# The last four token tiles' picks of the first two routing rounds, on GpSimd instead of VectorE

## The chip, the cores and the metric

The program runs on one core of a Trainium2 chip. The metric is the device time of one execution in microseconds, from the first instruction of the core to its end. TensorE (PE in the rows) multiplies matrices, VectorE (DVE), ScalarE (ACT) and GpSimd (POOL) work on elements, and SyncE (SP) issues most of the large transfers.

## The reference, cut to what matters

Three stages follow each other: a windowed attention with sink keys, a mixture of experts with a capacity, and a dense feed-forward. The change lies in the second. Cut to it:

```
N, D, E, F = (1536, 512, 8, 1024)
cap = N // E                                  # 192 tokens for each expert
logits = x @ w_gate
order = np.argsort(-logits.flatten())
for idx in order:                             # best (token, expert) pairs first
    tok, e = (int(idx) // E, int(idx) % E)
    if assigned[tok] >= 0 or counts[e] >= cap:
        continue
    assigned[tok] = e
    counts[e] += 1
for e in range(E):
    mask = assigned == e
    h = np.maximum(x[mask] @ w1[e], 0.0)
    out[mask] = h @ w2[e]
```

After it every token runs through `g = max(x @ w_in, 0) + alpha * min(x @ w_in, 0)` and `g @ w_out`.

## The kernel before

The 1536 tokens lie as 12 tiles of 128 (`NT` is 12). The sequential loop of the reference is worked off in eight routing rounds. Each round finds the next expert that becomes full, with all 192 of its tokens. Round `r` goes like this. PE and VectorE rank the keys (`beats`, `ties`, `count`); VectorE takes the tokens in front of the filling one (`assign`), which raises `round_done`; PE counts for each token how many stand before it (`before_and_loads`); VectorE works out in `fill_expert` which expert is full and, for each token, its number among that expert's tokens (`slot`, one column for each token tile, 0 for a token that is not in it).

Then come the picks, the step of this study. For each token tile `c` one instruction writes `in_slot[:, c, :]`, 128 partitions by 192 numbers of 16 bits: 1 where `slot_iota` (1 to 192) equals the token's slot, else 0. It reads `slot_iota` as its tensor and `slot[:, c]` as one number for each partition. PE multiplies these one-hot tiles with the token numbers (`pick_tokens`): for each tile one matmul for 128 of the 192 slots and one for the other 64, 24 matmuls of one column in all. They are issued in two parts, `PARTS`, first tiles 0 to 7 (16 matmuls), then tiles 8 to 11 (8 matmuls), and each part waits for the picks of its tiles (`picks_ready`). `token_numbers` copies the result into `tok_next` on VectorE, and GpSimd gathers the 192 token rows with two indirect transfers (`gather`).

The order on each engine is the order in which its program is written. Around the picks it is:

- Round 0: nothing of the experts runs yet. VectorE does `assign(0)`, `fill_expert(0)`, 12 picks, `token_numbers(0)`, and then the key of the next round (`wanted_key(1)`). PE issues multiplications of zeros between its routing steps (`keep_clock`, 14 of them before `pick_tokens(0)` and 4 behind it), and then `rows(1, c)`, which waits for the key. The copies of ScalarE and the comparisons of VectorE of round 1 hang on that.
- Round 1: PE multiplies expert 0's tokens at the same time. `pick_tokens(1)` stands behind the second of the four output blocks of that expert. VectorE does 8 picks, `y_rest(0, 0)`, 4 picks, `token_numbers(1)`, `wanted_key(2)`.
- GpSimd has nothing to do between the attention's end and `gather(0)`, and nothing between `gather(0)` and `gather(1)`, other than one memset of a single number (`awake`), which waits for the first part of the picks. After that it splits `w_in` for the feed-forward (`split_wi`, `wi_lo`).

Later rounds (2 to 7) run beside the feed-forward or the experts and aren't touched by the change, but for the threshold that PE waits for.

Of the kernel before, what the change touches and what calls it, by code (L numbers as in the profile page):

```python
# [22 lines left out]
ALU = mybir.AluOpType  # L23
ACT = mybir.ActivationFunctionType
AX = mybir.AxisListType.X
# [33 lines left out]
def program(nc, q_t, k_t, k_sink, v_rows, v_sink_d, wg_d, w1_d, w2_d, w_in_d, w_out_d, alpha_d, out, n_sink, window):  # L59
# [9 lines left out]
    with ctx:  # L69
        def sb(name, shape, dt=F32, at=None):  # L70
            return (at or ctx).enter_context(nc.sbuf_tensor(name, shape, dt))

        def sem(name):
            return ctx.enter_context(nc.semaphore(name))
# [13 lines left out]
        slot = sb("slot", [P, NT])  # L88
# [9 lines left out]
        slot_iota = sb("slot_iota", [P, CAP], F16)  # L98
# [49 lines left out]
        def in_turn(first, then):  # L148

            place = ExitStack()  # L150
            made = [sb(*a, at=place) for a in first]
            place.close()
            return made + [sb(*a) for a in then]
# [22 lines left out]
        in_slot, beats = in_turn([("in_slot", [P, NT, CAP], F16)], [("beats", [P, 3, N], BF16)])  # L176
# [13 lines left out]
        lack = sb("lack", [P, NT, E])  # L190
# [64 lines left out]
        round_done = sem("round_done")  # L255
# [6 lines left out]
        w1_loaded = [[sem(f"w1_loaded{e}_{n}") for n in range(2)] for e in range(2)]  # L262
        w2_loaded = [sem(f"w2_loaded{e}") for e in range(2)]
        picks_ready = sem("picks_ready")
        picked = sem("picked")
        tok_ready = sem("tok_ready")
        tok_moved = sem("tok_moved")
# [58 lines left out]
        PARTS = (range(0, 8), range(8, NT))  # L326
# [137 lines left out]
        def _(pool):  # L464
# [123 lines left out]
            def gather(r):  # L588

                if r >= 2:  # L590
                    pool.wait_ge(x_turned, TURNS * (r - 1))
                for k, (t, rows) in enumerate(ROWS[r % 2]):
                    n = TURNS * (r % 2) + k
                    pool.wait_ge(tok_ready, TURNS * r + k + 1)
                    nc.gpsimd.indirect_dma_start(
                        out=x_g[rows, t, :], out_offset=None, in_=x_dram[:, :],
                        in_offset=bass.IndirectOffsetOnAxis(ap=tok_next[0:rows.stop - rows.start, n:n + 1], axis=0),
                    ).then_inc(gathered[r % 2][k], 16)
# [5 lines left out]
                                        in1=wi_hi[:, f % 2, :, :].bitcast(F32), op=ALU.subtract)\  # L604
                  .then_inc(wi_split, 1)

            pool.wait_ge(picks_ready, 1)
            nc.gpsimd.memset(awake[:, :], 0.0)
            gather(0)
            gather(1)  # L610

            def group(j):
# [211 lines left out]
        def _(dve):  # L824
            chain = Chain(dve, dve_order)
# [177 lines left out]
            def first_filler(r):  # L1003
                dve.wait_ge(across_done, r + 1)
                chain.after(nc.vector.tensor_reduce(out=top[:, :], in_=ACROSS, axis=AX, op=ALU.min))
# [21 lines left out]
            def fill_expert(r):  # L1027

                e = r % 2
                dve.wait_ge(loads_counted, r + 1)
                chain.after(nc.vector.scalar_tensor_tensor(out=full_new[:, e, :], in0=LOADS, scalar=float(CAP),
                                                           in1=full[:, :], op0=ALU.is_ge, op1=ALU.subtract))
                nc.vector.tensor_tensor(out=numbered[:, :], in0=full_new[:, e, :], in1=expert_no[:, 0, :], op=ALU.mult)
                nc.vector.tensor_tensor(out=full[:, :], in0=full[:, :], in1=full_new[:, e, :], op=ALU.add)
                chain.after(nc.vector.tensor_tensor(out=lack[:, :, :], in0=assigned[:, :, :],
                                                    in1=full_new[:, e, :].unsqueeze(1).to_broadcast([P, NT, E]), op=ALU.mult))
                nc.vector.tensor_reduce(out=off[:, 0:1], in_=numbered[:, :], axis=AX, op=ALU.add)
                nc.vector.tensor_scalar(out=full_pen[:, :], in0=LOADS, scalar1=float(CAP), scalar2=-BIG,  # L1040
                                        op0=ALU.is_ge, op1=ALU.mult)
                chain.after(nc.vector.scalar_tensor_tensor(out=lack[:, :, :], in0=SLOTS, scalar=1.0, in1=lack[:, :, :],
                                                           op0=ALU.add, op1=ALU.mult))
                if r >= 2:
                    dve.wait_ge(w2_loaded[e], 16 * (r // 2))
                nc.vector.tensor_scalar(out=expert_of[e][:, :], in0=off[:, 0:1], scalar1=-1.0, scalar2=float(E),
                                        op0=ALU.mult, op1=ALU.add).then_inc(expert_known, 1)
                nc.vector.tensor_scalar(out=start_row[:, :, 0:E], in0=LOADS[0:1, :].unsqueeze(1).to_broadcast([1, NT, E]),
                                        scalar1=1.0 - CAP, scalar2=None, op0=ALU.add).then_inc(room_ready, 1)
                chain.after(nc.vector.tensor_reduce(out=slot[:, :], in_=lack[:, :, :], axis=AX, op=ALU.add))  # L1050

            def picks(r, tiles):

                for c in tiles:
                    last = nc.vector.tensor_scalar(out=in_slot[:, c, :], in0=slot_iota[:, :],
                                                   scalar1=slot[:, c:c + 1], scalar2=None, op0=ALU.is_equal)
                last.then_inc(picks_ready, 1)
# [34 lines left out]
            first_filler(0)  # L1092
            assign(0)
            fill_expert(0)
            for tiles in PARTS:
                picks(0, tiles)
            token_numbers(0)
            wanted_key(1)
            wanted(1)
# [2 lines left out]
            def experts(j):  # L1102

                r = 2 * j
                if j == 0:
                    fillers(1)
                    first_filler(1)
                    assign(1)
                    fill_expert(1)
                    picks(1, PARTS[0])  # L1110
                    y_rest(0, 0)
                    picks(1, PARTS[1])
                    token_numbers(1)
                    wanted_key(2)
                    y_rest(0, 1)
                    wanted(2)
                    move_tokens(0)
                    y_rest(0, 2)
                    y_rest(0, 3)
                    for c in range(3):  # L1120
                        compare(2, c)
                elif j < NG - 1:
                    first_filler(r + 1)
                    assign(r + 1)
                    fill_expert(r + 1)
                    wanted_key(r + 2)
                    for tiles in PARTS:
                        picks(r + 1, tiles)
                    token_numbers(r + 1)
                    wanted(r + 2)  # L1130
                    y_rest(r, 0)
                    y_rest(r, 1)
                    compare(r + 2, 0)
                    compare(r + 2, 1)
                    y_rest(r, 2)
                    compare(r + 2, 2)
                    y_rest(r, 3)
                    move_tokens(j)
                else:
                    for m in range(DC):  # L1140
                        y_rest(r, m)
                    move_tokens(j)
                    for m in range(DC):
                        y_rest(r + 1, m)
                    return
                for c in range(3, 9):
                    compare(r + 2, c)
                y_rest(r + 1, 0)
                for c in range(9, 11):
                    compare(r + 2, c)  # L1150
                y_rest(r + 1, 1)
                compare(r + 2, 11)
                y_rest(r + 1, 2)
                fillers(r + 2)
                first_filler(r + 2)
                y_rest(r + 1, 3)
# [71 lines left out]
        def _(pe):  # L1228
# [222 lines left out]
            def pick_tokens(r):  # L1451


                sets = sorted(enumerate(ROWS[r % 2]), key=lambda s: s[1][1].start - s[1][1].stop)
                for part, tiles in enumerate(PARTS if r < 2 else (range(NT),)):
                    pe.wait_ge(picks_ready, len(PARTS) * r + (part + 1 if r < 2 else len(PARTS)))
                    for k, (t, rows) in sets:
                        n, count = TURNS * (r % 2) + k, rows.stop - rows.start
                        at = t * P + rows.start - r % 2 * CAP
                        for c in tiles:  # L1460
                            last = nc.tensor.matmul(PICKED[0:count, n:n + 1], in_slot[:, c, at:at + count], token_no[:, c:c + 1],  # L1461
                                                    start=(c == 0 and count == P), stop=(c == NT - 1), skip_group_check=True)
                last.then_inc(picked, 1)
# [244 lines left out]
```

## Time and profile before

| what | us |
|---|---|
| median of 3 runs | 640.17 |
| lowest and highest of them | 639.58, 641.13 |
| span of the profiled execution | 638.6 |
| PE busy in it | 619.2 (97%) |
| VectorE busy | 418.5 (66%) |
| ScalarE busy | 306.8 (48%) |
| GpSimd busy | 197.0 (31%) |

The span runs from the first to the last instruction of one execution; the median is 1.6 us above it, since the whole execution has a little in front of and behind its instructions. A time of the form 135.26 is a place in the span. In the timeline an entry "x12" spans the first start to the last end of twelve instructions that follow each other.

### The profile page before, as it was taken

How to read it: one execution, taken by the hardware profiler on the slowest of the kernel's cores; microseconds unless marked ns; L12 is line 12 of the kernel's file. 1: busy time of each engine (PE TensorE's matmuls, PEld its weight loads, DVE VectorE, ACT ScalarE, POOL GpSimd, SP SyncE). 2: the span in 40 equal slices, each digit the busy share in tenths (PEclk: the TensorE clock that was granted, in tenths of full speed). 3: DMA queues.
4: the chain of work that ended last, by engine and by line, in shares of the span. 5: the costliest groups of instructions: out<-in, count | busy, mean ns of one | idle time of the engine just before them, and what ended most of it. 6: DMA issues, size and time to landing. Idle time of an engine off the chain costs nothing.

```text
span 638.6 us, 12935 instructions
## 1 busy us (share of the span) xinstructions
PE 619.2 (97%) x4949; PEld 556.5 (87%) x4954; DVE 418.5 (66%) x1156; ACT 306.8 (48%) x716; POOL 197.0 (31%) x211
## 2 busy tenths in 40 slices
PE   8899999889999999999999999999999999999996
PEld 4788898759899888899999888999989889999995
DVE  8788787978566979854669798438587420035552
ACT  5878784511132665532236554322465642346663
POOL 5988880010111442111113331111234410113331
PEclk9999999989999999999999999999999999999999
DMA  7477764525350143027102510370016620000001
GB/s 259 150 264 265 260 203 139 210 92 200 113 227 1 67 141 133 2 84 255 52 2 73 201 66 3 116 272 1 2 67 222 240 81 19 1 1 1 1 1 50
DMA packets 31221, 72.37 MB, mean 113 GB/s; under 512 B 2876, under 2 KB 2936, under 8 KB 31160
## 3 DMA queue, kind: packets, MB, share of 16 engines
q1 hardware_dynamic: 27232, 60.69, 27.0%
q0 software_dynamic: 1984, 6.29, 3.0%
q10 hardware_dynamic: 1944, 4.56, 2.0%
q8 instruction: 40, 0.66, 0.4%
q14 instruction: 21, 0.17, 0.1%
HBM read 65.22 MB, written 6.32 MB: 112 GB/s over the span
## 4 chain that ended last, share of the span: by engine, by line
PE 76%; DVE 3%; DMA 1%; issue 0%; POOLq 0%; ACT 0%; POOL 0%; DVEq 0%
PE bank L1602 21%; PE bank L1617 21%; PE bank L1514 14%; PE bank L1505 13%; PE bank L1392 3%; DVE beats L971 1%; DMA rank_row<-key_row 1%; PE bank L1461 1%; PE bank L1483 1%; DVE beats L942 1%; PE bank L1445 0%; PE bank L1233 0%; DVE ties L984 0%; PE bank L1394 0%; PE bank L1438 0%
## 5 line engine op out<-in xcount | busy, mean ns | idle before, releaser
L603 POOL TENSOR_TENSOR wi_lo<-w_in,wi_hi 128x512 fp32r<-128x512 f32 x64 | 89.5, 1401 | 274.2 <-ACT wi_hi L744 274.2
L942 DVE TENSOR_SCALAR beats<-rank_row,key 128x512 bf16<-128x512 f32 (+11 forms) x144 | 91.3, 655 | 12.4 <-PE bank L1394 12.4
L1617 PE MATMUL bank<-wo_lo,g_hi 128*128 128x512 f32 x192 | 76.0, 396 | 0.0
L1617 PE MATMUL bank<-wo_hi,g_lo 128*128 128x512 f32 x192 | 75.7, 394 | 0.0
L1617 PE MATMUL bank<-wo_hi,g_hi 128*128 128x512 f32 x192 | 75.5, 393 | 0.0
L1215 DVE SCALAR_TENSOR_TENSOR g<-bank,g_neg 128x384 f32<-128x384 f32 x64 | 35.5, 554 | 52.9 <-ACT g_neg L796 52.9
L794 ACT ACTIVATE g_neg<-bank 128x384 f32<-128x384 f32 x64 | 31.4, 491 | 79.9 <-PE bank L1602 79.1
L668 ACT ACTIVATE prob<-neg_s,neg_max 128x260 f32<-128x260 f32 x96 | 48.9, 510 | 19.1 <-DVE neg_max L853 17.7
L1602 PE MATMUL bank<-y_hi,wi_hi 128*128 128x384 f32 x256 | 57.9, 347 | 0.0
L770 ACT ACTIVATE h_t<-bank 128x192 f32<-128x192 f32 x64 | 21.2, 331 | 74.3 <-PE bank L1505 74.3
L1602 PE MATMUL bank<-y_lo,wi_hi 128*128 128x384 f32 x256 | 55.2, 336 | 0.0
L1602 PE MATMUL bank<-y_hi,wi_lo 128*128 128x384 f32 x256 | 54.7, 334 | 0.0
L1205 DVE TENSOR_TENSOR g_lo<-g,g_hi 128x384 fp32r<-128x384 f32 x64 | 44.4, 694 | 14.7 <-ACT g_hi L801 14.5
L1083 DVE TENSOR_TENSOR y_lo<-bank,y_hi 128x192 fp32r<-128x192 f32 x32 | 11.3, 354 | 60.3 <-ACT y_hi L781 60.2
L1514 PE MATMUL bank<-h_t,w_b 128*128 128x192 f32 x256 | 47.7, 334 | 0.0
L781 ACT CAST y_hi<-bank 128x192 fp32r<-128x192 f32 x32 | 10.2, 319 | 77.5 <-PE bank L1514 77.5
L1602 PEld LDWEIGHTS bank<-y_hi,wi_hi 128*128 128x128 f32 x256 | 44.1, 188 | 3.4 <-ACT y_hi L781 0.2
L1602 PEld LDWEIGHTS bank<-y_lo,wi_hi 128*128 128x128 f32 x256 | 46.2, 188 | 0.0
L1505 PE MATMUL bank<-x_gt,w_b 128*128 128x192 f32 x256 | 45.3, 330 | 0.7 <-ACT x_gt L760 0.7
L1199 DVE TENSOR_TENSOR wo_lo<-w_out,wo_hi 128x512 fp32r<-128x512 f32 x64 | 45.8, 715 | 0.0
L1602 PEld LDWEIGHTS bank<-y_hi,wi_lo 128*128 128x128 f32 x256 | 45.3, 188 | 0.0
L801 ACT CAST g_hi<-g 128x384 fp32r<-128x384 f32 x64 | 32.9, 513 | 24.9 <-DVE g L1215 20.2
(180 smaller groups left out, 1364.6 us busy)
## 6 DMA issues: line engine op xcount, KB each, us to landing
w_a<-moe_w SPq DMA_DIRECT2D x8, 1024.0 KB, 5.0
w_a<-moe_w SPq DMA_DIRECT2D x4, 2048.0 KB, 11.4
w_b<-moe_w SPq DMA_DIRECT2D x8, 1024.0 KB, 5.1
w_b<-moe_w SPq DMA_DIRECT2D x4, 2048.0 KB, 10.5
k_raw<-k_t SPq DMA_DIRECT2D x11, 512.0 KB, 4.8
q_raw<-q_t SPq DMA_DIRECT2D x11, 512.0 KB, 3.9
w_in<-moe_w_in SPq DMA_DIRECT2D x8, 512.0 KB, 5.2
w_out<-moe_w_out SPq DMA_DIRECT2D x8, 512.0 KB, 5.2
```

What stands on the lines that cost most here:

```text
L603: nc.gpsimd.tensor_tensor(out=wi_lo[:, f % 2, :, :], in0=w_in[:, :, f * P:(f + 1) * P], in1=wi_hi[:, f % 2, :, :].bitcast(F32), op=ALU.sub ...
L668: nc.scalar.activation(prob[b][:, h, :], neg_s[:, h % 4, :], ACT.Exp, bias=neg_max[b][:, h:h + 1], scale=-1.0, accum_out=p_sum[b][:, h, 0: ...
L794: nc.scalar.activation(g_neg[:, :], UP_BANK[f % 2][:, 0:GS], ACT.Relu, scale=-1.0).then_inc(neg_turned, 1)
L801: nc.scalar.copy(g_hi[:, f % 3, :], g[:, f % 2, :]).then_inc(g_hi_done, 1)
L942: return nc.vector.tensor_scalar(out=beats[:, c % 3, lo:hi], in0=rank_row[:, lo:hi], scalar1=key[:, c:c + 1], scalar2=None, op0=op)
L1199: nc.vector.tensor_tensor(out=wo_lo[:, f % 2, :], in0=w_out[:, f, :], in1=wo_hi[:, f % 2, :].bitcast(F32), op=ALU.subtract).then_inc(wo_sp ...
L1205: nc.vector.tensor_tensor(out=g_lo[:, f % 3, :], in0=g[:, f % 2, :], in1=g_hi[:, f % 3, :].bitcast(F32), op=ALU.subtract).then_inc(g_split, 1)
L1215: nc.vector.scalar_tensor_tensor(out=g[:, f % 2, :], in0=u, scalar=0.0, in1=g_neg[:, :], op0=ALU.max, op1=ALU.add).then_inc(g_ready, 1)
L1505: last = nc.tensor.matmul(into, w1[e][:, c, k * P:(k + 1) * P], x_gt[e][:, c, :], start=(c == 0), stop=(c == DC - 1))
L1514: last = nc.tensor.matmul(into, w2[e][:, f, m * P:(m + 1) * P], h_t[e][:, f, :], start=(f == 0), stop=(f == EC - 1))
L1602: last = nc.tensor.matmul(UP_BANK[f % 2][:, 0:GS], w[:, f % 2, c, :], y[:, c, :], start=(n == 0), stop=(n == len(passes) - 1))
L1617: last = nc.tensor.matmul(DOWN_BANK[t][:, :], a[:, f % 3, t * P:(t + 1) * P], w[:, f % 2, :], start=(f == 0 and n == 0), stop=(f == FC - 1 ...
```

## The change

In rounds 0 and 1 the picks of tiles 8 to 11 move from VectorE to GpSimd (`last_picks`). GpSimd waits there for a new semaphore `slot_ready`, which VectorE raises when `slot` is written, and it raises `pool_picks_ready` behind its fourth pick; PE's second part waits for that one. In round 1 GpSimd also waits until PE has read the `in_slot` of round 0. The `awake` memset waits for `round_done` of round 0 instead of the first picks.

```diff
-            pool.wait_ge(picks_ready, 1)
+            def last_picks(r):
+
+                pool.wait_ge(slot_ready, r + 1)
+                if r:
+                    pool.wait_ge(picked, r)
+                for c in PARTS[1]:
+                    last = nc.gpsimd.tensor_scalar(out=in_slot[:, c, :], in0=slot_iota[:, :],
+                                                   scalar1=slot[:, c:c + 1], scalar2=None, op0=ALU.is_equal)
+                last.then_inc(pool_picks_ready, 1)
+
+            pool.wait_ge(round_done, 1)
             nc.gpsimd.memset(awake[:, :], 0.0)
+            last_picks(0)
             gather(0)
+            last_picks(1)
             gather(1)
...
-                chain.after(nc.vector.tensor_reduce(out=slot[:, :], in_=lack[:, :, :], axis=AX, op=ALU.add))
+                slots = nc.vector.tensor_reduce(out=slot[:, :], in_=lack[:, :, :], axis=AX, op=ALU.add)
+                slots.then_inc(slot_ready, 1)
+                dve.wait_ge(slot_ready, r + 1)
...
-            for tiles in PARTS:
-                picks(0, tiles)
+            picks(0, PARTS[0])
...
                     picks(1, PARTS[0])
                     y_rest(0, 0)
-                    picks(1, PARTS[1])
...
-                    pe.wait_ge(picks_ready, len(PARTS) * r + (part + 1 if r < 2 else len(PARTS)))
+                    if r < 2 and part:
+                        pe.wait_ge(pool_picks_ready, r + 1)
+                    else:
+                        pe.wait_ge(picks_ready, r + 1 if r < 2 else len(PARTS) * r - 2 + len(PARTS))
```

The order of VectorE in round 1, before and then in the change. `slot` is the last step of `fill_expert(1)`, `in_slot` are the picks, `y_lo` is `y_rest`, `tok_next` is `token_numbers(1)`, and `lm`, `best` and `key` are the next round's key.

```order
L1050 TENSOR_REDUCE slot<-lack 128x12
L1055 TENSOR_SCALAR in_slot<-slot_iota,slot 128x192 [waits dve_order]
L1055 TENSOR_SCALAR in_slot<-slot_iota,slot 128x192 x7
L1083 TENSOR_TENSOR y_lo<-bank,y_hi 128x192 [waits y_hi_done]
L1055 TENSOR_SCALAR in_slot<-slot_iota,slot 128x192 x4
L1068 CAST tok_next<-bank 64x1 [waits picked]
```

```order
L1063 TENSOR_REDUCE slot<-lack 128x12
L1070 TENSOR_SCALAR in_slot<-slot_iota,slot 128x192 [waits slot_ready]
L1070 TENSOR_SCALAR in_slot<-slot_iota,slot 128x192 x7
L1098 TENSOR_TENSOR y_lo<-bank,y_hi 128x192 [waits y_hi_done]
L1083 CAST tok_next<-bank 64x1 [waits picked]
```

Four picks have left VectorE behind `y_lo`; its other instructions keep their order. In round 0 the same four are gone from one row of twelve.

The order of GpSimd from the end of the attention to the first `wi_lo`, before and then in the change. `x_g` are the gathers, two for each round.

```order
L608 MEMSET awake 1x1 [waits picks_ready,x_stored1,x_stored0]
L595 DMA x_g<-x_rows,tok_next 128x512 [waits tok_ready]
L595 DMA x_g<-x_rows,tok_next 64x512 [waits tok_ready] x2
L595 DMA x_g<-x_rows,tok_next 128x512 [waits tok_ready]
L603 TENSOR_TENSOR wi_lo<-w_in,wi_hi 128x512 [waits wi_hi_done] x9
```

```order
L619 MEMSET awake 1x1 [waits round_done,x_stored1,x_stored0]
L614 TENSOR_SCALAR in_slot<-slot_iota,slot 128x192 [waits slot_ready]
L614 TENSOR_SCALAR in_slot<-slot_iota,slot 128x192 x3
L596 DMA x_g<-x_rows,tok_next 128x512 [waits tok_ready]
L596 DMA x_g<-x_rows,tok_next 64x512 [waits tok_ready]
L614 TENSOR_SCALAR in_slot<-slot_iota,slot 128x192 [waits picked,slot_ready]
L614 TENSOR_SCALAR in_slot<-slot_iota,slot 128x192 x3
L596 DMA x_g<-x_rows,tok_next 64x512 [waits tok_ready]
```

Four picks now stand in front of each pair of gathers. PE's order is the same as before; only the semaphore of its second part differs.

## Rows read from the trace of the kernel before

**Rows 1.** The page's chain that ended last: shares of the span by engine
```profile
PE 76%; DVE 3%; DMA 1%; issue 0%; POOLq 0%; ACT 0%; POOL 0%; DVEq 0%
```
**Rows 2.** Timeline, round 0: start us, us, engine line op out<-in xcount [idle before]
```profile
133.40 3.18 PE L1233 MATMUL bank<-zeros 128*128 128x512 bf16 x14
...
135.26 2.24 DVE L1055 TENSOR_SCALAR in_slot<-slot_iota,slot 128x192 f16<-128x192 f16 x12
...
136.84 1.19 PE L1461 MATMUL bank<-token_no,in_slot 128*128 128x1 f16 x24 [0.25 <-DVE in_slot L1055]
...
138.18 0.81 PE L1233 MATMUL bank<-zeros 128*128 128x512 bf16 x3 [0.16 <-issue]
...
138.76 0.17 DVE L925 TENSOR_TENSOR key<-best,cap_val 128x12 f32<-128x12 f32 x1
```
**Rows 3.** The chain of waits, round 0: start us, us, what
```profile
135.26 1.53 DVE in_slot L1055 x8
...
137.55 0.47 PE bank L1461 x8
...
138.99 1.17 PE bank L1374 x8
```
**Rows 4.** Timeline, round 1
```profile
164.60 1.52 DVE L1055 TENSOR_SCALAR in_slot<-slot_iota,slot 128x192 f16<-128x192 f16 x8
...
166.31 0.80 DVE L1055 TENSOR_SCALAR in_slot<-slot_iota,slot 128x192 f16<-128x192 f16 x4
...
166.72 1.08 PE L1461 MATMUL bank<-token_no,in_slot 128*128 128x1 f16 x24
...
167.84 0.21 DVE L1068 CAST tok_next<-bank 64x1 uint32<-64x1 f32 x2 [0.73 <-PE bank L1461]
```
**Rows 5.** The chain of waits, round 1
```profile
166.88 0.92 PE bank L1461 x24
167.80 2.80 PE bank L1514 x16
```
**Rows 6.** Timeline of GpSimd and VectorE in the first feed-forward
```profile
220.90 1.29 POOL L603 TENSOR_TENSOR wi_lo<-w_in,wi_hi 128x512 fp32r<-128x512 f32 x1 [3.71 <-ACT wi_hi L744]
221.07 2.44 DVE L1055 TENSOR_SCALAR in_slot<-slot_iota,slot 128x192 f16<-128x192 f16 x8
...
224.97 1.44 DVE L1055 TENSOR_SCALAR in_slot<-slot_iota,slot 128x192 f16<-128x192 f16 x4
...
242.75 1.57 POOL L603 TENSOR_TENSOR wi_lo<-w_in,wi_hi 128x512 fp32r<-128x512 f32 x1 [3.78 <-ACT wi_hi L744]
242.77 0.41 DVE L942 TENSOR_SCALAR beats<-rank_row,key 128x384 bf16<-128x384 f32 x1
...
243.09 1.38 DVE L951 SCALAR_TENSOR_TENSOR ties<-rank_row,key,tri_after 128x128 bf16<-128x128 f32 x1
```
**Rows 7.** The same two engines in front of the first feed-forward
```profile
189.94 4.02 POOL L603 TENSOR_TENSOR wi_lo<-w_in,wi_hi 128x512 fp32r<-128x512 f32 x2 [19.50 <-ACT wi_hi L744]
```
**Rows 8.** GpSimd's groups by shape: line, operation, xcount | busy us, mean ns
```profile
L367 POOL TENSOR_TENSOR k_lo<-k_raw,k_hi 128x1024 fp32r<-128x1024 f32 x10 | 23.8, 2382 | 6.3 <-ACT k_hi L355 5.8
...
L531 POOL COPY sink_p<-prob 128x32 f32<-128x32 f32 x36 | 6.1, 211 | 8.4 <-ACT prob L668 7.9
...
L496 POOL COPY turn_gate<-ident 128x512 f32<-128x512 f32 x1 | 0.6, 608 | 0.0
...
L468 POOL TENSOR_SCALAR_AFFINE_SELECT ident<-ident 128x128 f32<-128x128 f32 x1 | 0.3, 294 | 0.1
```
**Rows 9.** Timeline: three packing copies of GpSimd in a row
```profile
103.48 0.51 POOL L531 COPY sink_p<-prob 128x32 f32<-128x32 f32 x3 [7.03 <-ACT prob L668]
```
**Rows 10.** Stages: us, then PE, PEld, DVE, ACT, POOL busy (x), PEclk, DMA
```profile
128.00:129.00 1.00, 0.66 (x16) 0.48 (x14) 1.00 (x5) 0.30 (x1) 0.00 (x0) 1.00 0.07 16
...
130.00:131.00 1.00, 0.92 (x3) 0.37 (x3) 0.72 (x4) 0.00 (x0) 0.00 (x0) 0.50 0.00 0
```
**Rows 11.** Timeline of PE: multiplications of zeros in a row at that clock
```profile
130.08 1.49 PE L1233 MATMUL bank<-zeros 128*128 128x512 bf16 x3 [0.24 <-issue]
```

More of the change, by code:

```diff
@@ L264, in program @@
         picks_ready = sem("picks_ready")
+        slot_ready, pool_picks_ready = sem("slot_ready"), sem("pool_picks_ready")
         picked = sem("picked")
```

## Prediction

> **What bounds the kernel now.** I read the page's chain first: three quarters of the span end in PE [rows 1], and VectorE holds the chain only where PE has nothing to multiply. So what the picks are worth depends on where they stand. The next views are the timeline and the chain of waits at the two places.
>
> In round 0 the picks are on the chain. VectorE makes twelve from 135.26 to 137.50, one every 0.18 us ((2.24 - 1.52) / 4 from [rows 2, 4]). PE's last filler starts its run at 133.40 and is over at 136.58, so PE waits for the eighth pick, begins at 136.84 and is done at 138.03 [rows 2]. Its second part begins at 137.55, just behind VectorE's last pick at 137.50 [rows 3]. Behind it come the key of round 1 at 138.76 [rows 2] and PE's spreading of it at 138.99 [rows 3].
>
> In round 1 the chain is PE all the way: it comes to the picks out of expert 0's multiplications, the first pick matmul starts at 166.72, and it goes on with the expert at 167.80 [rows 4, 5]. VectorE's eighth pick is done at 166.12 and its twelfth at 167.11 [rows 4], both before PE asks for them, and VectorE then waits 0.73 us for PE [rows 4]. The picks cost nothing there.
>
> **What the change can give.** In round 0 PE's second part need no longer wait for VectorE's last four picks. What that wait costs now is seen by comparing the 24 matmuls of round 0, 1.19 us, with the same 24 in round 1, where nothing holds them, 1.08 us [rows 2, 4]: 0.11 us. The four picks themselves take 0.72 us of VectorE, but 0.61 of it lies beside PE's first sixteen matmuls. In round 1 the gain is nothing, for VectorE waits for PE behind them anyway. The new wait of GpSimd (for `slot_ready`) has nothing queued behind it but the gathers, and they need PE's result first. The earlier `awake` memset, the semaphore on `slot` in place of the old one and SP's queue (the expert's weights hang on the gathers and shift with them) I cost at nothing.
>
> **What a pick costs GpSimd.** No row shows it. From below: copies, one input and no comparison, take 211 ns for 32 numbers and 608 for 512 [rows 8], 0.83 ns a number, so 0.34 us for 192. The instruction nearest in kind, the affine select with its comparison, takes 294 ns for 128 numbers [rows 8]; 64 more at the copies' slope make 0.35. From above: the two-input subtraction takes 1.29 us for 512 when nothing disturbs it [rows 6] and 2.38 for 1024 [rows 8], 2.13 ns a number, so 0.61 us for 192. I take 0.50, a little above the middle, because a pick fetches one number for each partition besides its row and then compares. Three short copies in a row take 0.51 us while each takes 0.21 [rows 9], so instructions that follow each other start 0.06 earlier than the last one ends: a pick every 0.44 us (0.28 to 0.55). Four of them side by side with VectorE would then be ready at about 135.35 + 1.76 = 137.1, in time.
>
> **What it costs VectorE.** This is the term that decides. The same VectorE picks run beside GpSimd's `wi_lo` in the feed-forward. Eight of them issued at 221.07, while a GpSimd instruction runs from 220.90 to 222.19, take 2.44 us instead of 1.52 [rows 4, 6]: 0.92 lost of the 1.12 that were left of it. Four issued at 224.97 take 1.44 instead of 0.80, 0.64 lost, again beside a `wi_lo` [rows 4, 6]. VectorE does nothing until GpSimd is nearly through (0.2 us before its recorded end), then goes on at its old pace. The other way round it holds too: the GpSimd instruction at 242.75 meets a comparison that VectorE issued at 242.77 and takes 1.57 us instead of 1.29, and the next VectorE instruction, issued at 243.09, takes 1.38 and ends 0.15 us behind GpSimd's [rows 6]. So a GpSimd instruction gets in behind the VectorE instruction that runs, and shuts out the next one.
>
> This is a rule of the Trainium skill, page "SBUF — State Buffer", section "Who interferes with whom": VectorE's fast modes for one-input instructions and any GpSimd instruction share one pair of ports, held for the whole instruction. By that rule, the trace agrees: 0.92 us of blocked picks. It speaks against the change, whose two lists of picks would take turns instead of running side by side.
>
> Applied to four GpSimd picks that start with VectorE's eight: VectorE does one pick in each gap, so four of its picks go at GpSimd's pace (0.44) and four at its own (0.18). Its eight take 4 x (0.44 - 0.18) = 1.04 us longer (0.40 to 1.48).
>
> **The sum.** Round 0: the eighth pick and with it all that follows moves by 1.04, and 0.11 comes back from the second part, which GpSimd has ready: +0.93 (0.29 to 1.37). PE, the key, the gathers and the first expert shift together, since all start from the same result. Round 1: the eighth pick is done at 166.12 + 1.04 = 167.16, PE sees it 0.04 later (as in round 0, 136.79 to 136.84 by [rows 3] and [rows 2]), at 167.20 instead of 166.72: +0.48 (nothing to 0.92). That PE time is on the chain [rows 5]. Together +1.41 us (0.3 to 2.3). The profiled execution would go from 638.6 to 640.0; it stands 1.6 under the median, and I carry the difference over to the median: 640.17 + 1.41 = 641.6.
>
> For the middle value the skill's page "GPSIMD Engine Reference", section "3.1 Elementwise — side-by-side cycle accounting", gives some 1.8 cycles a number for a good one-input loop; with the copies' fixed part of 0.18 us that would be an estimate of 0.47 us a pick and a sum of 1.2. No run here shows it.
>
> **The rivals.**
>
> *They do run side by side (not slower).* If a short 16-bit pick on GpSimd held the ports only for a small part of its time, VectorE's eight would end at 136.79 as now and only the 0.11 would be left: 640.1, no change to be measured. For it: the blocking rows are all of instructions of 1.3 us, and VectorE got back in 0.2 us before the end of each; of a pick of 0.35 us little more than half would then block. It decides if GpSimd's pick is at the bottom of its bounds or below. Against it: the rows show no partial overlap otherwise.
>
> *VectorE keeps the ports.* Two `wi_lo` that take 2.5 us alone took 4.02 at 189.94, while VectorE was in a dense run of comparisons [rows 7]. If GpSimd is kept out until VectorE's eight are through at 136.79, its four end at 136.79 + 1.76 + 0.06 = 138.61, and PE's last eight matmuls (0.47, [rows 3]) follow 0.04 later: 139.12 instead of 138.03, +1.1. Round 1: 166.12 + 1.82 + 0.04 + 0.47 = 168.45 instead of 167.80, +0.65. Together 641.9.
>
> *TensorE's clock falls as well.* In round 0 PE's wait from 136.58 grows from a quarter to over one microsecond, and behind it come only matmuls of one column. The stretch around 130 shows what may follow: at 128 to 129 PE ran narrow matmuls with gaps at a granted clock of 1.00 (2.4 GHz), at 130 to 131 the clock was 0.50 (1.2 GHz) [rows 10], and three multiplications of zeros took 1.49 us where they take 0.81 at 2.4 GHz [rows 11, 2]. If it falls behind the picks, the four fillers take about 0.9 longer than the key they cover, and the key's first eight matmuls, 1.17 us [rows 3], up to 0.9 more: +1.8, so 643.4.
>
> *GpSimd's pick is dearer than every row.* At 1.0 us each the eight picks of VectorE take 4 x (0.94 - 0.18) = 3.0 longer: +2.9 in round 0, and in round 1 166.12 + 3.04 + 0.04 - 166.72 = +2.5: 645.6.
>
> **How the numbers follow.** Taking turns at 0.34 to 0.61 us a pick: 0.46, from 640.5 to 642.5. Side by side: 0.18. VectorE first: 0.12. The clock on top: 0.17. A dear pick: 0.07. About 0.2% (1.3 us) is what a measurement of this kernel can tell from no change, which puts the bound at 641.45. Of the first case some six tenths lie above it, of VectorE first most, of the last two all: slower 0.59, the same 0.38. Nothing in the trace gives back more than 0.11 us, so faster has only 0.03, for a chance of the measurement. The range reaches from the side-by-side case to above the case with the clock: 640.0 to 644.0.
>
> **What would show it.** In the profile after: VectorE's eight picks of round 0 at 2.3 to 3.0 us instead of 1.52, single ones above 0.26; GpSimd's four at 0.34 to 0.61 each; PE's first pick matmul at 137.2 to 138.3 instead of 136.84; all 24 in 1.08; in round 1 PE's first at up to 167.6. If VectorE's eight stay at 1.52 and GpSimd's four end behind 137.4, the second rival is true; if both are short, the first. A granted clock of 0.50 between 138 and 142 is the third. The prediction is wrong if VectorE isn't held up, or if what follows the picks in round 0 had slack that I haven't seen.

## The result, and the profile after

| | before | the change |
|---|---|---|
| median of 12 runs, us | 640.16 | 642.83 |
| lowest to highest | 639.21 to 641.91 | 641.35 to 644.14 |
| span of the profiled execution | 638.6 | 642.0 |
| mean granted clock of TensorE in it | 0.997 | 0.987 |

The ratio is 1.0034, 95% interval 1.0025 to 1.0043: slower by 2.2 us (1.6 to 2.8). The direction and the range were right. The forecast of 641.6 was 1.2 us below the median, and its +1.4 us was 0.8 below what the ratio gives. The reason was only half right, and that is what the rest is about.

The timeline of the changed kernel in round 0, which answers to [rows 2] (start us, us, engine, line, operation; GpSimd's picks are L614, VectorE's L1070, PE's matmuls L1477):

```profile
136.58 2.12 DVE L1070 TENSOR_SCALAR in_slot<-slot_iota,slot 128x192 f16<-128x192 f16 x8
136.65 3.06 POOL L614 TENSOR_SCALAR in_slot<-slot_iota,slot 128x192 f16<-128x192 f16 x4 [2.15 <-DVE slot L1063]
...
138.76 0.69 PE L1477 MATMUL bank<-token_no,in_slot 128*128 128x1 f16 x16 [0.85 <-DVE in_slot L1070]
...
139.77 0.47 PE L1477 MATMUL bank<-token_no,in_slot 128*128 128x1 f16 x8 [0.32 <-POOL in_slot L614]
...
140.40 1.14 PE L1246 MATMUL bank<-zeros 128*128 128x512 bf16 x3 [0.16 <-issue]
...
140.98 0.17 DVE L938 TENSOR_TENSOR key<-best,cap_val 128x12 f32<-128x12 f32 x1
```

The forecast's first sign is there: VectorE's eight picks take 2.12 us instead of 1.52. The last thing that PE waits for is another one: GpSimd's four take 3.06, and the second part begins at 139.77, 0.32 us idle with GpSimd named as its releaser. The chain of waits says the same, in round 0 and in round 1 (start us, us, what):

```profile
136.65 3.08 POOL in_slot L614 x4
...
139.77 0.47 PE bank L1477 x8
```
```profile
167.94 3.08 POOL in_slot L614 x4
...
171.06 0.47 PE bank L1477 x8
```

VectorE's picks, which headed [rows 3], are no longer in it. The forms of the two lines, minimum, median and maximum in ns:

```profile
L614 POOL TENSOR_SCALAR in_slot<-slot_iota,slot x8: 750/751/848, 136.6 to 170.3; 128x192 f16<-128x192 f16 x8
```
```profile
L1070 DVE TENSOR_SCALAR in_slot<-slot_iota,slot x8: 271/422/439, 136.6 to 138.3; 128x192 f16<-128x192 f16 x8
```

A GpSimd pick costs 0.75 us, more than the 0.61 that I had taken for the upper bound, and it costs that too where VectorE has long been done. Five of VectorE's eight picks take 0.42 to 0.44 instead of 0.26.

Behind round 0's picks the clock of TensorE falls, which it did not do there before. The stages of the changed kernel (us, then busy time of PE, PEld, DVE, ACT and POOL, then the granted clock):

```profile
136.60:138.70 2.10, 1.31 (x7) 0.39 (x4) 2.10 (x8) 0.00 (x0) 2.05 (x3) 1.00 0.22 23
140.70:144.20 3.50, 3.50 (x17) 3.01 (x16) 2.00 (x9) 0.58 (x1) 2.11 (x2) 0.51 0.64 214
```

From 140.7 on the clock stands at its lower level, 1.2 GHz, for 3.4 us. Ahead of that PE waited, then ran the one-column matmuls. Three multiplications of zeros take 1.14 us (0.81 in [rows 2]), and the 24 matmuls that spread the key take 4.21 instead of 2.94 (timeline of the changed kernel, then of the kernel before):

```profile
141.33 4.21 PE L1387 MATMUL bank<-ident,key 128*128 128x128 f32 x24
```
```profile
138.99 2.94 PE L1374 MATMUL bank<-ident,key 128*128 128x128 f32 x24
```

**The 3.4 us of the two spans, by stage.** The stretch up to round 0's first pick takes 136.58 instead of 135.26, +1.32. It holds nothing of the change: this execution had one more fall of the clock during the attention, as this stage shows for the changed kernel and then for the one before.

```profile
17.00:30.00 13.00, 10.86 (x77) 8.98 (x76) 6.73 (x28) 9.26 (x28) 10.93 (x12) 0.74 0.45 162
```
```profile
17.00:30.00 13.00, 10.19 (x94) 8.69 (x92) 8.24 (x35) 10.89 (x36) 11.98 (x13) 1.00 0.49 180
```

From that pick to the first transposing of expert 0's tokens it takes 11.79 instead of 9.85, +1.94. Then come 19.50 us in both. From round 1's first pick to the transposing of expert 1's tokens it takes 9.96 instead of 9.50, +0.46. The rest is 464.13 instead of 464.47, and lies between 464.10 and 464.52 in all the kernels below. So the change itself costs 2.40 us in this execution, in the two places where it was made, and nothing of it is given back.

### The profile page after: what moved, and what is told of

Same layout as the page of the kernel before. It is cut to its first block, busy times and chain, and to the rows that moved or that the text cites. A ratio compares the mean times of both kernels' runs of the same rounds, so it can differ in the third digit from the quotient of the medians.

```text
span 642.0 us, 12936 instructions
## 1 busy us (share of the span) xinstructions
PE 622.1 (97%) x4949; PEld 559.8 (87%) x4954; DVE 419.0 (65%) x1148; ACT 306.8 (48%) x716; POOL 201.4 (31%) x219
## 4 chain that ended last, share of the span: by engine, by line
PE 77%; DVE 2%; POOL 1%; issue 0%; POOLq 0%; ACT 0%; DVEq 0%
PE bank L1618 21%; PE bank L1633 21%; PE bank L1521 13%; PE bank L1530 13%; PE bank L1405 3%; DVE beats L984 1%; PE bank L1499 1%; POOL in_slot L614 1%; PE bank L1246 1%; PE bank L1477 1%; PE bank L1387 1%; PE bank L1458 0%; PE bank L1402 0%; DVE ties L997 0%; PE bank L1407 0%
## 5 line engine op out<-in xcount | busy, mean ns | idle before, releaser
L604 POOL TENSOR_TENSOR wi_lo<-w_in,wi_hi 128x512 fp32r<-128x512 f32 x64 | 88.0, 1377 | 275.4 <-ACT wi_hi L757 275.4
L1521 PE MATMUL bank<-x_gt,w_a 128*128 128x192 f32 x256 | 44.8, 329 | 0.0
```

Of the source, the lines that this page charges most:

```text
L604: nc.gpsimd.tensor_tensor(out=wi_lo[:, f % 2, :, :], in0=w_in[:, :, f * P:(f + 1) * P], in1=wi_hi[:, f % 2, :, :].bitcast(F32), op=ALU.sub ...
L1521: last = nc.tensor.matmul(into, w1[e][:, c, k * P:(k + 1) * P], x_gt[e][:, c, :], start=(c == 0), stop=(c == DC - 1))
```

## The experiments

Two theories stood against each other. **A**: GpSimd's own price of 0.75 us a pick, with a fall of the clock behind it. **B**: the forecast's, that VectorE is shut out while GpSimd picks. The table holds what the traces of all kernels but the two with short forms showed, in us. Each row of it is one profiled execution. A filler is one of PE's multiplications of zeros. "Picks" runs from VectorE's first pick to the end of PE's last pick matmul; "stage" runs from that pick to the next transposing of gathered tokens on PE; then comes where the clock stood at 0.50 behind the picks. Ratios are against the kernel before, measured beside each kernel. Last pieces has one transposing record missing in round 1, and the work behind it bears out its 9.50.

| kernel | picks 0 | stage 0 | clock 0.50 at | picks 1 | stage 1 | ratio (95%) |
|---|---|---|---|---|---|---|
| before | 2.76 | 9.85 | no | 3.20 | 9.50 | 1 |
| the change | 3.66 | 11.79 | 140.7 to 144.2 | 3.66 | 9.96 | 1.0034 (1.0025 to 1.0043) |
| the change again | 3.66 | 11.81 | 139.6 to 143.0 | 3.67 | 9.97 | 1.0037 (1.0023 to 1.0050) |
| round 0 only | 3.88 | 12.03 | 139.3 to 142.7 | 3.19 | 9.50 | 1.0025 (1.0015 to 1.0036) |
| round 1 only | 2.76 | 9.85 | no | 3.88 | 10.18 | 1.0008 (0.9998 to 1.0018) |
| three fillers | 3.88 | 10.96 | no | 3.66 | 9.96 | 1.0021 (1.0011 to 1.0032) |
| four fillers | 3.65 | 10.74 | 148.3 to 151.7 | 3.66 | 9.97 | 1.0039 (1.0023 to 1.0054) |
| spare picks | 3.26 | 11.62 | 139.8 to 143.2 | 3.96 | 10.26 | 1.0022 (1.0011 to 1.0034) |
| two tiles | 3.09 | 10.17 | no | 3.20 | 9.50 | 1.0007 (0.9994 to 1.0020) |
| last pieces | 2.77 | 9.85 | no | 3.19 | 9.50 | 1.0002 (0.9989 to 1.0014) |

In stage 0 every kernel is the kernel before plus what its picks take longer, plus the fall if there is one: 11.79 - 9.85 = 1.94 = 0.90 + 1.04; 12.03 - 9.85 = 2.18 = 1.12 + 1.06; 10.96 - 9.85 = 1.11 against 1.12 without a fall. With the spare picks the fall begins 1.0 us behind the last pick matmul instead of 0.3 to 0.6, lies wholly over the spreading of the key, and costs more: 11.62 - 9.85 = 1.77 = 0.50 + 1.27.

**Round 0 only.**

```diff
             last_picks(0)
             gather(0)
-            last_picks(1)
             gather(1)
...
                     y_rest(0, 0)
+                    picks(1, PARTS[1])
...
```

> The change in round 0 alone; round 1's last four picks stay on VectorE. Theory A (read from the changed kernel's trace): the loss is GpSimd's own price, 0.75 us a pick, for which PE's second part waits (picks from first start to PE's last matmul 3.66 us instead of 2.77, +0.89), and a fall of the clock behind it (+1.05); round 1 adds only 0.46. So this one is slower than before by 1.9 us, ratio 1.0030, and shows a granted clock of 0.50 around 141. Theory B (the forecast's: VectorE shut out by GpSimd's picks carries the loss, no clock effect): +0.9, ratio 1.0014, with the clock at 1.00 there.

The ratio was 1.0025 (+1.6 us) and the trace shows the fall:

```profile
139.00:140.00 1.00, 1.00 (x4) 0.33 (x5) 0.91 (x6) 0.00 (x0) 0.52 (x1) 0.65 1.06 414
140.00:141.00 1.00, 1.00 (x6) 0.98 (x5) 0.86 (x5) 0.00 (x0) 0.69 (x2) 0.50 0.23 88
```

A's 1.0030 lies in the interval and B's 1.0014 just below it. Most of the loss is in round 0. The picks took 3.88 here and not the 3.66 that A had: GpSimd's first two took 0.93 and 0.90, and VectorE's eight only 1.94.

**Round 1 only.**

```diff
-            last_picks(0)
             gather(0)
             last_picks(1)
...
+            for tiles in PARTS:
+                picks(0, tiles)
-            picks(0, PARTS[0])
...
```

> The change in round 1 alone; round 0 as before. Both theories: PE waits beside expert 0 for GpSimd's fourth pick and ends its 24 matmuls 3.66 us behind the first pick instead of 3.20: +0.46 us, ratio 1.0007, hardly to be told from no change. No fall of the clock that the kernel before doesn't have. If the ratio is above 1.002, round 1 has a price that neither theory holds.

The ratio was 1.0008, which can't be told from no change or from the 0.68 us that its stage shows. PE reaches the second part and waits for GpSimd (timeline):

```profile
167.99 0.68 PE L1477 MATMUL bank<-token_no,in_slot 128*128 128x1 f16 x16
...
169.29 0.47 PE L1477 MATMUL bank<-token_no,in_slot 128*128 128x1 f16 x8 [0.62 <-POOL in_slot L614]
```

The first part starts 2.11 us behind the first pick, as before: VectorE's delay alone (1.95 for eight) would have cost nothing in this execution. The whole price is GpSimd's fourth pick. This is the clearest evidence for A. An estimate for round 0 agrees: four picks at the 0.75 us that they take in the changed kernel once VectorE is done, begun 0.07 behind VectorE's first, then 0.04 and PE's 0.47, make 3.58 us, so 0.82 of the 0.90 would be there without any slowing of either engine.

**Spare picks.** The kernel before; GpSimd makes the same picks once more for nobody.

```diff
+            def spare_copy(r):
+                pool.wait_ge(slot_ready, r + 1)
+                for c in PARTS[1]:
+                    last = nc.gpsimd.tensor_scalar(out=o_sb[...].bitcast(F16), in0=slot_iota[:, :],
+                                                   scalar1=slot[:, c:c + 1], scalar2=None, op0=ALU.is_equal)
...
+            spare_copy(0)
             gather(0)
+            spare_copy(1)
             gather(1)
...
```

> The kernel before, in which GpSimd makes the picks of tiles 8 to 11 of rounds 0 and 1 a second time into a place that nobody reads, while VectorE makes all twelve and PE waits for VectorE alone. This leaves the contention of the two engines and takes away the wait for GpSimd. Theory A (a GpSimd pick of 0.75 us shuts VectorE out for about 0.2 us): VectorE's twelve take some 0.7 longer than 2.24, ratio 1.001 without a fall of the clock, each GpSimd pick 0.75 as when alone. Theory B (held for the whole instruction): VectorE's twelve take 2.24 + 4 x (0.74 - 0.18) = 4.5 us, +2.2 us, ratio 1.0035.

The timeline of round 0:

```profile
135.51 2.73 DVE L1070 TENSOR_SCALAR in_slot<-slot_iota,slot 128x192 f16<-128x192 f16 x12
135.57 3.30 POOL L612 TENSOR_SCALAR o_sb<-slot_iota,slot 128x192 f16<-128x192 f16 x4 [2.15 <-DVE slot L1063]
```

VectorE's twelve take 2.73 us instead of 2.24, +0.49, where B said 4.5. The timeline of round 1:

```profile
166.63 2.13 DVE L1070 TENSOR_SCALAR in_slot<-slot_iota,slot 128x192 f16<-128x192 f16 x8
...
168.95 1.12 DVE L1070 TENSOR_SCALAR in_slot<-slot_iota,slot 128x192 f16<-128x192 f16 x4
...
170.12 0.47 PE L1476 MATMUL bank<-token_no,in_slot 128*128 128x1 f16 x8 [0.61 <-DVE in_slot L1070]
```

The eight lose 0.61 there and the four 0.32. So four GpSimd picks cost VectorE 0.49 to 0.93 us, 0.12 to 0.23 for each of them, not their whole length of 0.75 to 0.93. Contention as the forecast sized it falls. It is not nothing either: with nobody waiting for GpSimd the picks of round 0 end 0.50 late and those of round 1 0.76, since VectorE's last four picks still have to come and PE waits for them. The clock fell behind round 0's picks here too, which neither theory had expected. The ratio of 1.0022 (+1.4 us) lies above A's 1.001 and below the 2.5 us that this execution's two stages lose; whether the clock falls in every execution of this kernel isn't known.

**Two tiles on GpSimd.** VectorE makes 8 and then 2 picks, GpSimd 2, in both rounds, and PE's second part waits for both engines.

```diff
-                for c in PARTS[1]:
+                for c in (10, 11):
...
             picks(0, PARTS[0])
+            picks(0, range(8, 10))
...
```

> The changed kernel with only tiles 10 and 11 on GpSimd; VectorE makes 8 and then 2 picks in both rounds, and PE's second part waits for both engines. Theory A (the loss is GpSimd's 0.75 us a pick, with VectorE losing about 0.15 us for each): GpSimd is done 1.6 us behind the first pick and no longer waited for; VectorE's eighth ends at 1.82 instead of 1.52, PE's last matmul at about 3.0 instead of 2.76 in round 0 (+0.2) and as before in round 1; no fall of the clock. Ratio 1.0004, not to be told from no change, and no gain either. Theory C (the clock falls wherever PE waits longer than before): the same with 1.05 us on top, ratio 1.002.

```profile
135.38 2.17 DVE L1070 TENSOR_SCALAR in_slot<-slot_iota,slot 128x192 f16<-128x192 f16 x10
135.45 1.81 POOL L614 TENSOR_SCALAR in_slot<-slot_iota,slot 128x192 f16<-128x192 f16 x2 [2.40 <-DVE slot L1063]
...
137.38 1.09 PE L1478 MATMUL bank<-token_no,in_slot 128*128 128x1 f16 x24
```

GpSimd is now done before VectorE, PE's 24 matmuls run through in 1.09, and the picks of round 0 still end at 3.09 instead of 2.76, since the eighth pick, for which PE waits first, is 0.42 late. That is somewhat above the 3.0 expected. Round 1 costs nothing and the clock stays up in this execution. The ratio of 1.0007 is not to be told from no change. This split doesn't pay either: it wins back the 0.11 us of the second part's wait and loses 0.42 at the eighth pick.

**Short forms on GpSimd.** Twice the kernel before, in which GpSimd issues short instructions behind round 1's gathers into a place that nobody reads. Each ran once.

```diff
             gather(1)
+            pool.wait_ge(y_copied, DC)
...
+            for n in range(3):
+                ts(out=f16(), in0=slot_iota[:, :], scalar1=slot[:, n:n + 1], scalar2=None, op0=ALU.is_equal)
+            for n in range(2):
+                ts(out=f16(96), in0=slot_iota[:, 0:96], scalar1=slot[:, n:n + 1], scalar2=None, op0=ALU.is_equal)
...
```

> The kernel before with fifteen short instructions of GpSimd into a place that nobody reads, issued behind round 1's gathers while VectorE is idle (it waits there for the keys' transfer): the pick as in the change (192 numbers of 16 bits), the pick of 96 numbers, the pick against a constant instead of a number for each partition, the pick of 96 numbers of 32 bits, a multiplication by a constant, a subtraction of two 16-bit rows, and a copy. If the comparison is what costs 0.75 us, the multiplication and the copy are under 0.4 and the constant pick is at 0.75; if it is the number for each partition, the constant pick is under 0.5; if it is the 16-bit type, the copy and multiplication are dear too and 96 numbers of 32 bits cost under 0.3; if it is a fixed price, 96 numbers cost nearly what 192 do.

> As the first kernel of short forms, in another order, since VectorE's comparisons began before the multiplication's turn came there: three multiplications of 192 16-bit numbers by a constant, two subtractions of a number for each partition, two subtractions of two rows, two copies and one pick, on GpSimd into a place that nobody reads while VectorE is idle. If the comparison costs the 0.75 us, the multiplication and the subtraction are under 0.5; if it is this kind of instruction (one row, one or two numbers), they are at 0.69 and 0.75 as well. The two-row subtraction should be near 0.5 and the copy near 0.39.

The groups of the first kernel while VectorE was idle, then of the second (line, operation, shape, xcount | busy us, mean ns):

```profile
L628 POOL TENSOR_SCALAR o_sb<-slot_iota,slot 128x192 f16<-128x192 f16 x3 | 2.3, 764 | 3.7 <-DVE y_lo L1117 3.7
L632 POOL TENSOR_SCALAR o_sb<-slot_iota 128x192 f16<-128x192 f16 x2 | 1.4, 690 | 0.1
L634 POOL TENSOR_SCALAR o_sb<-expert_no,slot 128x96 f32<-128x96 f32 x2 | 1.0, 520 | 0.1
L630 POOL TENSOR_SCALAR o_sb<-slot_iota,slot 128x96 f16<-128x96 f16 x2 | 1.0, 510 | 0.0
```
```profile
L628 POOL TENSOR_SCALAR o_sb<-slot_iota 128x192 f16<-128x192 f16 x3 | 2.0, 691 | 3.7 <-DVE y_lo L1112 3.7
L630 POOL TENSOR_SCALAR o_sb<-slot_iota,slot 128x192 f16<-128x192 f16 x2 | 1.5, 758 | 0.0
L632 POOL TENSOR_TENSOR o_sb<-slot_iota 128x192 f16<-128x192 f16 x2 | 1.0, 495 | 0.0
...
L634 POOL COPY o_sb<-slot_iota 128x192 f16<-128x192 f16 x2 | 0.6, 333 | 0.0
```

Alone, the pick takes 0.76 us (L628 of the first). It isn't the comparison: multiplying by a constant takes 0.69 (L628 of the second), the same as comparing with a constant, 0.69 (L632 of the first). It isn't the 16-bit type: 96 numbers take 0.52 in 32 bits and 0.51 in 16. The number for each partition adds 0.07. It is the kind of instruction, one row with one number: from 0.51 for 96 to 0.75 for 192 it costs 2.5 ns a number and 0.27 fixed. The copy at 0.33 is the forecast's lower bound of 0.34 nearly to the digit. The two-input subtraction, from which the upper bound of 0.61 came, takes 0.50 here, and an instruction with one row less to read takes half as much again.

The first kernel's two multiplications met VectorE's long comparisons, and they show that GpSimd can be held up as well: 2.90 us for the two that take 1.4 alone (timeline).

```profile
180.19 1.29 DVE L974 TENSOR_SCALAR beats<-rank_row,key 128x1536 bf16<-128x1536 f32 x2
180.26 2.90 POOL L636 TENSOR_SCALAR o_sb<-slot_iota 128x192 f16<-128x192 f16 x2
```

**Fillers against the fall.** Three more multiplications of zeros in front of the picks; then those and one between the parts; and the changed kernel itself, measured beside the second.

```diff
-            keep_clock(14, spare)
+            keep_clock(17, spare)
...
+                    if r == 0 and part:
+                        keep_clock(1, spare)
```

> The changed kernel with 17 multiplications of zeros instead of 14 in front of round 0's picks, which fill 0.65 of the 0.85 us in which PE waits for VectorE's eighth pick. Theory A: the clock doesn't fall behind the picks, the 1.05 us come back, and the kernel is slower than before by 1.4 us (ratio 1.0021) instead of 2.2 to 2.4. Theory B: nothing changes against the changed kernel, ratio 1.0034. If the clock falls all the same, fillers there don't keep it, and the ratio stays at 1.0034 too; the trace tells the two apart.

> The changed kernel itself, once more, beside the next one on the same chip. Theory A (+0.9 to +1.1 in round 0, +0.5 in round 1, and a fall of the clock behind round 0's picks, +1.05): ratio 1.0035 to 1.004, the clock at 0.50 somewhere between 139 and 145 in the profile. Without the clock's part it would be 1.0023.

> The changed kernel with 17 multiplications of zeros instead of 14 in front of round 0's picks and one more between the two parts, so that PE's two new waits there are nearly filled. Theory A: no fall of the clock behind the picks, ratio 1.0022, about 1 us under the changed kernel of the same call. If the clock's fall costs nothing in the end, both have the same ratio.

With three fillers the profiled execution keeps its clock through the stage that falls without them:

```profile
140.00:141.00 1.00, 1.00 (x10) 1.00 (x11) 0.90 (x5) 0.00 (x0) 0.69 (x2) 1.00 0.14 51
141.00:142.00 1.00, 1.00 (x11) 1.00 (x11) 0.59 (x4) 0.66 (x2) 0.77 (x1) 1.00 0.65 180
```

PE gets 21 matmuls through there; the changed kernel got 17 through in the 3.5 us shown above. The span was 639.6 and the ratio 1.0021, as A said, though its interval overlaps that of the change. The trace of round 0 only is the best one to compare with: its picks take the same 3.88, the clock was low from 129.0 to 132.6 in both executions, and only the one without the fillers has the second fall. The changed kernel again gave 1.0037, as A said. But with four fillers the ratio was 1.0039, and A's 1.0022 fell. In its trace the clock held at 140 to 144 and went down a little later, behind the narrow matmuls of round 1's first counts and under expert 0's first multiplications.

```profile
140.00:144.00 4.00, 4.00 (x31) 3.35 (x31) 3.45 (x14) 1.87 (x4) 1.67 (x2) 1.00 0.49 148
148.30:151.70 3.40, 3.40 (x24) 3.23 (x23) 3.21 (x8) 0.33 (x1) 0.00 (x0) 0.50 1.01 378
```

That fall costs 1.55 us: the stretch between the stages takes 21.05 instead of 19.50. Whether the fillers moved the fall there isn't shown. It is one execution, and its earlier falls lie elsewhere than in the changed kernel's (120.8 to 124.4 and 131.2 to 134.6). The timed executions can't tell either. Those with three fillers took 641.3 to 641.9 us at a mean granted clock of 0.994 or more and 642.5 to 643.5 at 0.990 or 0.991, but the kernel before beside them has the same two groups: 639.3 to 641.5 at 0.994 or more, 640.8 to 642.0 at 0.991 or less. What is shown is that three fillers kept the clock in one execution and that four brought no gain by the ratio.

**Last pieces.** The kernel before, with fillers also beside the last four pieces of round 0's count.

```diff
-                        if n < len(PIECES) - 4 and n >= 4:
+                        if n >= 4:
```

> The kernel before with one more multiplication of zeros beside each of the last four pieces of round 0's count, where the clock falls in every profile so far (129 to 133 us). It tells what a fall of the clock costs in this stretch, without any of the change. If fillers there keep the clock, the 3.4 us at 0.50 go and with them about 1 us, ratio 0.9985; if they come too late or delay the count, no change or +0.3 us, with the fall still in the trace.

The fall around 130 that every other profile has is gone (this kernel, then the kernel before):

```profile
128.00:134.00 6.00, 4.64 (x49) 2.45 (x49) 4.11 (x21) 0.30 (x1) 0.00 (x0) 1.00 0.01 3
```
```profile
128.00:134.00 6.00, 4.76 (x44) 2.60 (x44) 3.72 (x18) 0.30 (x1) 0.00 (x0) 0.72 0.01 3
```

Round 0's first pick then starts at 134.84 instead of 135.26, 0.4 us earlier, not 1, for VectorE sets the pace there. Both executions stand within 0.01 us of each other at round 0's key (113.54 and 113.55), so the 0.4 is what this fall costs. In the timed runs even that doesn't show (1.0002, 0.9989 to 1.0014). The price of a fall differs with the work under it: 0.4 us here, 1.0 to 1.3 behind the picks, 1.55 under an expert's multiplications. No kernel here beats the one before.

## Why the prediction came out as it did

**Right: what bounds the kernel, and what there was to gain.** The picks stand on the chain in round 0 and beside the expert in round 1, and everything behind them shifts with them: the 19.50 us between the stages and the rest of the span are the same in both. The gain of 0.11 us at most was right too. Once the second part isn't held, as with two tiles, the 24 matmuls take 1.09.

**Wrong: the price of a GpSimd pick.** Bounded at 0.34 to 0.61 us and taken as 0.50, it measures 0.75. The upper bound was the step that failed: I took the two-input subtraction for it and gave no reason why a pick can't cost more. The runs show that it does (0.75 against 0.50 for the subtraction of two rows of 192), so the kind of instruction decides, not the number of rows read. I had given a dear pick 0.07, priced at 1.0 us.

**Wrong: the size of VectorE's loss.** Its mechanism is there, but a term of 1.04 us for eight picks measures 0.60, and 0.42 where GpSimd's first two picks were slower. I carried over from the 1.3 us subtraction that a GpSimd instruction holds VectorE for nearly its whole length [rows 6]. Of a pick's 0.75 us it holds only 0.12 to 0.23. The rule of the Trainium skill, page "SBUF — State Buffer", section "Who interferes with whom", that the loser is blocked for the whole instruction, fits the subtraction (0.92 lost of the 1.12 left) and not the pick: there the measurement decides.

**So the sum was right for a reason that wasn't.** Round 0's picks cost 0.90 where I said 0.93, and round 1's 0.46 where I said 0.48. In both the forecast had VectorE's eighth pick ending late and GpSimd's four ready in time. In fact VectorE's eighth was 0.6 late and PE then waited a second time, for GpSimd's fourth. Two errors, a pick too cheap and a block too long, cancelled within 0.03 us, and that is luck: in two other executions the same change of round 0's picks cost 1.12. Only the experiments told the two apart: alone in round 1, GpSimd's fourth pick is what PE waits for, and with the spare picks VectorE's twelve lose 0.49 and 0.93, not 2.2.

**Right as a rival: the clock.** It had a chance of 0.17 and a price of 1.8 on top. It came in both profiled executions of the change and costs 1.04 us. I priced the fillers and the first eight matmuls of the key as if each waited for the other; part of it lies beside VectorE's comparisons. The forecast held nothing for it, and it is the main part of what its sum lacks. With it the parts make 0.90 + 1.04 + 0.46 = 2.40 against 2.2 measured by the ratio. It had a claim to be in the forecast itself, since the change lengthens a wait of PE where its neighbours are narrow matmuls, and [rows 10] showed a fall behind such a stretch. In the profiles the clock fell behind round 0's picks in the four executions in which PE stood idle for 0.67 us or more in front of them (the change twice, round 0 only, spare picks), and in none of the others. That this wait is the cause is likely from that and from the three fillers, and no more than likely: where the earlier falls lie also differs from one execution to the next.

**The other rivals.** Side by side is false: VectorE loses 0.60. VectorE keeping the ports is false too: GpSimd's first pick starts with VectorE's first and takes 0.85, only 0.1 more than alone. Only beside VectorE's long comparisons was GpSimd held up much, as the first kernel of short forms shows.

**Open:** why a pick of GpSimd shuts VectorE out for only a part of its time while the subtraction does so for nearly all. There are two ways in which the eight and the four interleave: GpSimd's first pick takes 0.85 and VectorE's eight 2.12, or GpSimd's first two take 0.93 and 0.90 and VectorE's eight 1.94 (GpSimd's four end 3.13 or 3.36 behind VectorE's first). Nothing here tells what decides it. How often the clock falls behind the picks over many executions isn't known; the mean clocks don't tell where it fell.

## What to carry to other kernels

Before a step goes to an idle engine, price it there by the same kind of instruction in the trace; if there is none, the nearest other kinds aren't bounds, and one short kernel that issues the form in an idle stretch measures it. Then compare with what the step delays: here 0.72 us of VectorE's work lay almost wholly beside PE's matmuls, so 0.11 us was to be had for 3.0 us of GpSimd. And where PE waits among narrow matmuls, a longer wait may cost a stretch at 1.2 GHz as well; fillers in the wait kept the clock in one execution here and brought no sure gain.

## What the runs showed of the hardware

- GpSimd, a row of 192 numbers of 16 bits compared with or multiplied by one number: 0.69 us with a constant, 0.75 with a number for each partition, and 0.51 for that with 96 numbers; the copy 0.33, the subtraction of two rows 0.50. VectorE makes the same pick every 0.18 us.
- The two engines disturb each other less with this form than with the 1.3 us subtraction: eight VectorE picks lose 0.42 to 0.60 us beside it, where single ones take 0.42 to 0.44 instead of 0.26. VectorE's comparisons of 1536 numbers hold GpSimd up more: two multiplications took 2.90 us beside them instead of 1.4.
- What a fall of TensorE's clock to 1.2 GHz costs goes by what runs under it: 0.4 us around 130, 1.0 at 140.7 to 144.2 and 1.3 at 139.8 to 143.2 with the spare picks, 1.55 at 148.3 to 151.7.
